# Expert stage: the gathered rows turned by a transposing DMA from the second tile on

## The reference

```python
def _moe2_ref(x, w_gate, w_output_gate, w1, w2):      # N=1792 tokens, D=768, E=8, F=1024
    logits = x @ w_gate
    e_idx = np.argmax(logits, axis=1)
    ...                                               # gate_w: softmax weight of the chosen expert
    for e in range(E):
        mask = e_idx == e
        h = np.maximum(x[mask] @ w1[e], 0.0)
        ye = h @ w2[e]
        out[mask] = gate_w[mask, None] * eom[mask, e, None] * ye
```

## Time and profile before

| | |
|---|---|
| median of 3 runs | 1143.07 us |
| the profiled execution, its own time | 1139.88 us |
| its span, first to last instruction | 1138.1 us |
| PE busy | 1100.3 us, 97% |
| DVE busy | 594.7 us, 52% |
| ACT busy | 425.9 us, 37% |
| POOL busy | 256.5 us, 23% |
| mean granted TensorE clock | 0.990 |
| DMA | 104.11 MB, mean 91 GB/s |

### The profile page before, as it was taken

The page is one execution under the profiler, slowest core; times in us unless marked ns, Lnnn a source line. Parts: engine busy times, 40 slices in busy tenths (PEclk is TensorE's granted clock), DMA queues, the critical chain, the costliest instruction groups (busy, mean ns, idle before and its releaser), DMA issues.

```text
span 1138.1 us, 17823 instructions
## 1 busy us (share of the span) xinstructions
PE 1100.3 (97%) x6617; PEld 573.3 (50%) x6618; DVE 594.7 (52%) x837; ACT 425.9 (37%) x631; POOL 256.5 (23%) x235
## 2 busy tenths in 40 slices
PE   7989999999999999999999999999898999999996
PEld 3434444444455555555555555556454555555554
DVE  7888888887433443333343300015656565556721
ACT  5768777777511111211111200001535253353510
POOL 4756767672200000000000000000211122112211
PEclk9999999999999999999999999999899999999999
DMA  5412222210121111111100501000848355366400
GB/s 144 122 49 62 61 65 58 66 25 17 60 67 56 56 55 55 55 55 55 55 28 1 195 28 41 28 32 23 296 163 319 118 211 206 108 217 225 142 20 18
DMA packets 71978, 104.11 MB, mean 91 GB/s; under 512 B 29310, under 2 KB 47870, under 8 KB 71920
## 3 DMA queue, kind: packets, MB, share of 16 engines
q1 hardware_dynamic: 63680, 89.84, 24.0%
q0 software_dynamic: 3120, 11.02, 2.7%
q10 hardware_dynamic: 5120, 2.48, 0.8%
HBM read 93.88 MB, written 13.76 MB: 95 GB/s over the span
## 4 chain that ended last, share of the span: by engine, by line
PE 87%; ACT 4%; DVE 4%; issue 2%; DMA 2%; ACTq 0%; POOL 0%; DVEq 0%; POOLq 0%; SPq 0%
PE ps L1434 29%; PE ps L1449 15%; PE ps L1528 12%; PE ps L1357 10%; PE ps L1506 7%; PE ps L1336 5%; PE ps L1316 2%; ACT arena L815 2%; DVE arena L1042 2%; PE ps L1348 2%; PE ps L1299 2%; PE ps L1338 1%; DMA arena<-in_moe_w 1%; PE ps L1515 1%; PE ps L1493 1%
## 5 line engine op out<-in xcount | busy, mean ns | idle before, releaser
L1434 PE MATMUL ps<-arena 128*128 128x448 f16 x1728 | 328.8, 352 | 0.0
L1434 PEld LDWEIGHTS ps<-arena 128*128 128x128 f16 x1728 | 168.1, 98 | 155.7
L1449 PE MATMUL ps<-arena 128*128 128x392 f16 (+1 forms) x1008 | 167.3, 329 | 2.4 <-DVE arena L1022 2.4
L1506 PE MATMUL ps<-arena 128*128 128x512 f16 x648 | 150.5, 388 | 5.6 <-DVE arena L1229 5.6
L1042 DVE SCALAR_TENSOR_TENSOR arena<-arena 128x768 f16<-128x768 f32 (+1 forms) x112 | 113.1, 1066 | 74.1 <-ACT arena L815 74.0
L1528 PE MATMUL ps<-arena 128*128 128x384 f16 x864 | 143.3, 326 | 4.0 <-DVE arena L1234 3.6
L1449 PEld LDWEIGHTS ps<-arena 128*128 (+1 forms) x1008 | 98.4, 98 | 70.4 <-DVE arena L1022 2.8
L1357 PE MATMUL ps<-arena 128*128 128x448 f32 x288 | 133.0, 573 | 0.0
L785 ACT ACTIVATE arena<-ps 128x448 f32<-128x448 f32 x48 | 26.1, 543 | 263.0 <-PE ps L1434 263.0
L1016 DVE SCALAR_TENSOR_TENSOR arena<-ps,arena 128x448 f32<-128x448 f32 x48 | 30.0, 624 | 176.0 <-PE ps L1434 96.1
L1528 PEld LDWEIGHTS ps<-arena 128*128 128x128 f16 x864 | 83.5, 98 | 58.6 <-issue 2.5
(11 more groups left out here) (170 smaller groups left out, 1078.7 us busy)
## 6 DMA issues: line engine op xcount, KB each, us to landing
arena<-in_moe_w SPq DMA_DIRECT2D x48, 512.0 KB, 6.3
arena<-in_moe_w SPq DMA_DIRECT2D x64, 384.0 KB, 3.9
arena<-in_qk SPq DMA_DIRECT2D x23, 448.0 KB, 3.5
y_parts<-arena SPq DMA_DIRECT2D x16, 384.0 KB, 2.3
arena<-in_v SPq DMA_DIRECT2D x48, 96.0 KB, 2.6
arena<-in_moe_w_out SPq DMA_DIRECT2D x12, 384.0 KB, 5.5
arena<-in_w_out_t SPq DMA_DIRECT2D x11, 384.0 KB, 3.1
arena<-in_moe_w_gate SPq DMA_DIRECT2D x10, 384.0 KB, 4.2
```

Source lines behind the costliest of these rows:

```text
L1434: last = nc.tensor.matmul(ps[:, 2 * (b % 2) + g, 0:S], up_w[s][:, g, c, wl], xt[:, b * KC + c, xl], start=(c == 0 and wl + xl == 0), stop= ...
L1449: last = nc.tensor.matmul(ps[:, 4 + 2 * s + h, 0:cols], gt[:, f, gl, bass.ds(t * 128, 128)], wo[:, f, wl, h, 0:cols], start=(f == 0 and gl ...
L1506: last = nc.tensor.matmul(ps[:, b, :], x_t[:, xl, c], w1_s[s][:, c, wl, b * 512:(b + 1) * 512], start=(c == 0 and xl + wl == 0), stop=(c = ...
```

## The change

From tile 1 on TensorE and VectorE no longer take part in turning the rows. ScalarE issues one transposing DMA for all twelve blocks, `x_rows` to `x_t`, after the second `Relu` of the tile before and ahead of `rows_done`. TensorE waits for that DMA (`x_turned`) before `up(g, 0)`, and the next gather waits for it too. Tile 0 is still turned by TensorE and VectorE.

```diff
 def gather(g):                                   # POOL
-    pool.wait_ge(rows_turned, turned)            # turned = g
+    pool.wait_ge(x_turned, turned)               # turned = 16 * g - 16
     nc.gpsimd.indirect_dma_start(out=x_rows, ...)
...
+def turn_rows(g):                                # ScalarE
+    read = 16 * g + 16 if isinstance(g, int) else act.to_reg(16 * g + 16)
+    act.wait_ge(route, ROUTE_DONE)
+    act.wait_ge(gathered, read)
+    act.dma_start_transpose(x_t.rearrange("p l c m -> p (l c) m"), x_rows).then_inc(x_turned, 16)
...
 def tile(e, s, before, first):                   # ScalarE, end of the loop over b
+                turn_rows(g + 1)
                 if is_at(g, 0):
                     split_high(e + 1, 1 - s, range(KC))
                 else:
                     rows_done(before)
...
 def tile(e, s, before, first):                   # VectorE, between the splits
-                rows_out(g + 1)
...
 def tile(e, s, before, first):                   # TensorE
     g = before + 1
-    pe.wait_ge(x_t_ready, g + 1)
+    if is_at(g, 0):
+        pe.wait_ge(first_x_ready, 1)
+    else:
+        pe.wait_ge(x_turned, 16 * g)
     up(e, s, g, 0, first)
     if not is_at(g, 0):
         turn_hidden(before, 0)
         turn_hidden(before, 1)
     up(e, s, g, 1, first)
-    turn_rows(g + 1)
```

More of the change, by code:

```diff
@@ L328, in attention_moe_moe_kernel @@
         rows_turned = sem("rows_turned")
-        x_t_ready = sem("x_t_ready")
+        first_x_ready = sem("first_x_ready")
+        x_turned = sem("x_turned")
         hid_sum = sem("hid_sum")
@@ L585, in gather @@
                 if not isinstance(g, int):
-                    read, turned, copied = pool.to_reg(16 * g), pool.to_reg(g), pool.to_reg(g + 1)
+                    read, turned, copied = pool.to_reg(16 * g), pool.to_reg(16 * g - 16), pool.to_reg(g + 1)
                     pool.wait_ge(route, ROUTE_DONE)
@@ L593, in gather @@
                     pool.wait_ge(gather_idx_ready, g + 1)
-                    wait(pool, rows_turned, g)
+                    wait(pool, rows_turned, min(g, 1))
+                    wait(pool, x_turned, 16 * (g - 1))
                     if is_at(g, 0):
@@ L1221, in _, with first_rows_out @@
             y_low(TT - 1, 1)
[L1223 to L1227, removed]
+            def first_rows_out():
+                dve.wait_ge(rows_turned, 1)
                 for l in range(2):
-                    last = nc.vector.tensor_copy(x_t[:, l].rearrange("p c m -> p (c m)"), ps[:, bank + l, :].bitcast(F16)[:, 0:DM])
-                last.then_inc(x_t_ready, 1)
+                    last = nc.vector.tensor_copy(x_t[:, l].rearrange("p c m -> p (c m)"), ps[:, 2 + l, :].bitcast(F16)[:, 0:DM])
+                last.then_inc(first_x_ready, 1)
             def turned_hidden(g, b):
@@ L1235, in turned_hidden @@
                     .then_inc(hid_t_ready, 1)
-            rows_out(0)
+            first_rows_out()
             split_low(0, 0, range(KC, PIECES))
@@ L1484, in _, with turn_first_rows @@
             down(TT - 1, 1, range(4, FC))
[L1487 to L1490, removed]
+            def turn_first_rows():
+                pe.wait_ge(gathered, 16)
                 for l in range(2):
                     for c in range(KC):
-                        last = nc.tensor.transpose(ps[:, bank + l, :].bitcast(F16)[:, c * 128:(c + 1) * 128],
+                        last = nc.tensor.transpose(ps[:, 2 + l, :].bitcast(F16)[:, c * 128:(c + 1) * 128],
                                                    x_rows[:, l * DM + c * 128:l * DM + (c + 1) * 128], ident)
@@ L1497, in up @@
             def up(e, s, g, b, first):
-                if b == 1:
-                    wait(pe, hid_ready, 2 * g)
+                wait(pe, hid_ready, 2 * g + b - 1)
                 for c in range(KC):
@@ L1550, in _ @@
             pe.wait_ge(route, ROUTE_DONE)
-            turn_rows(0)
+            turn_first_rows()
             over_experts(pe, tile)
```

## The result

The changed kernel is slower: 1161.65 us median (1160.39 to 1162.46, 4 runs) against 1142.9 us (4 runs), ratio 1.0166, 95% interval 1.0148 to 1.0183. The profiled execution has a span of 1158.6 us against 1138.1.

The account below looks back on a forecast made before the run. PE was taken as the bound, with 87% of the chain of waits. (D - 1.96) - 0.67 + (D + 0.1) - 6.0 = 2 D - 8.5 = +4.7 us at D = 6.6, median 1147.8 us; 8-in-10 range 1139.5 to 1195.

Parts of the forecast that it names:

- rival B: The DMA outlasts rows_down, so PE waits for x in every tile from 2 on: +53 us, 1196 us; chance 0.25.
- D: Time from when ScalarE may issue the transposing DMA until PE may go on; taken as 6.6 us, bounds 2.3 and 9.6.
- D hidden in ordinary tiles: In ordinary tiles rows_down covers the transposing DMA, with 7.0 to 7.2 us available, so PE does not wait for x.
- term of -6.0 us: Nine tiles (4, 5, 7, 9, 10, 12, 14, 16, 17) each gain PE's 0.67 us of turning x.
- Which work was on the path: Of PE's 12.1 us removed, ordinary tiles gain 0.67 us each; second tiles of experts 2 to 6 gain nothing.
- The form of the two odd places: Tiles 1 and 3 cannot hide the DMA: shifts of D - 1.96 = +4.6 us and D + 0.1 = +6.7 us.
- budget of 8.3: Cover in us for the DMA in the five second tiles; each us of D beyond it costs one there.
- Nothing but rows_done and the splits stand behind the issue: On ScalarE only rows_done and w2 splits follow the issue; rows_done waits 8.05 us for PE anyway, so issuing is free.
- No cost to others: No term for slowed transfers; weights landing later by sharing DMA engines was named only as a way to be wrong.
- C: The DMA's twelve blocks are served one after another, D is 17 us: +169 us, 1312 us; chance 0.10.
- A: Quick transfer: D between 2.3 and 4.2 us at tiles 1 and 3; 1139.2 us at D = 2.3; chance 0.21.
- estimate of 1.5 us of transfer: Transposing DMA's transfer by the skill's 261 GB/s, putting D near its lower bound in an idle stretch.

Follow-up runs that it names:

- no_turning: The kernel before with the transposes and copies of x left out from tile 1 on, nothing in their place: 1134.51 us, ratio 0.9917.
- pool_order: The changed kernel with POOL's copy of the scatter indices ahead of the gather that waits for the transposing DMA: 1161.87 us, ratio 1.0149.
- traffic_only: The kernel before plus 18 transposing DMAs of 384 KB between scratch buffers, whose result no engine needs: 1150.54 us, ratio 1.0072.
- small_packets: The changed kernel with ScalarE's DMA as a plain copy in 1536 pieces of 256 bytes, turning nothing: 1155.11 us, ratio 1.0102.
- early_tile3: The changed kernel, but in tile 2 ScalarE issues tile 3's DMA after eight w2 splits, ahead of six of w1: 1156.64 us, ratio 1.0123.

## Why the prediction was wrong

It had the direction, slower, and put the loss at 4.7 us; 18.8 us were measured. That 1161.65 us lies in the wide range is owed to rival B, for whose sake the range reached to 1195. The step that failed is "D hidden in ordinary tiles", with its term of -6.0 us.

- **Which work was on the path**: right. no_turning gave -8.6 us; ordinary tiles went to 16.5 us, and the second tiles' turning lay in the shadow of the chain over the splits. (36 copies are not 19.8 us of DVE, since all 38 are busy 19.3; nothing hangs on it.)
- **The form of the two odd places**: right, and they hold most of the loss, but not their sizes. Tile 1 had D = 6.4 against 6.6 taken. Its step grew by 5.8 us, not 4.6, since the gather itself landed 12.9 us after tile 0's start and not 11.6. The step after it grew by 0.5 us where 0.7 less was expected: the eighteen matmuls behind the longer pause took 6.94 us against 5.75, at a granted clock of 0.57 against 0.70, which I had counted at nothing. (In the other runs that wait for x there they took 5.4 to 6.8 us.) Tile 3 was released by the DMA 9.6 us after its issue, taken as 6.6. `rows_down` came at 887.07, 17.85 us after the earlier trace rows, where 10.7 was predicted: 2.8 from tiles 1 and 2, about 3.0 from D, and 1.4 from the wait for DVE behind the late `rows_done`.
- **"D hidden in ordinary tiles"**: this is the step that failed. I took one D for all tiles and named 9.6 only as a far bound that would hold everywhere. It did not hold everywhere, but in exactly the second tiles of experts 1 to 5 D was 9.3 to 10.7 us, beyond the budget of 8.3: the eight w2 splits free their buffers just before, so the load traffic is in the way. Between tiles 4 and 17 the term was -5.4 us and came out as +2.2. Of these 7.6 us, 5.1 are the waits for x ahead of tiles 7, 9, 12 and 14, and 1.4 are waits for DVE of 2.02 and 1.54 us in tiles 11 and 15 instead of 1.08; 0.8 are three ordinary steps of 16.7 or 16.8 us. The rule that each us beyond the budget costs one is roughly borne out: D of 9.3, 10.1 and 10.4 gave waits of 0.7, 1.5 and 1.7 us, and 10.7 only 1.2, since `rows_down` of that tile began 2.02 us late.
- **"Nothing but rows_done and the splits stand behind the issue"**: true of ScalarE, but POOL was read for its gathers only. The copy of the scatter indices stands behind the gather, and `rows_done` waits for it. I named what was queued behind the waiting instruction on one engine of two. What this cost the changed kernel is not known by itself, since pool_order shows no gain.
- **No cost to others**: I asked whether the weights would land later only as a way to be wrong. traffic_only puts it at some 3 to 5 us, an estimate, mostly at the awaited weights of tile 3.
- **Rivals**: B had the right mechanism for second tiles, and its +53 us was much too much since D was 3.7 to 6.4 us in twelve of the 18 tiles. The blocks are not served one after another, as C had it: alone the DMA takes 3.7 us, not 17. A's 2.3 us is not reached even by the plain copy, 2.6.
- The Trainium skill (DMA: Bandwidth & Descriptors, the table with the effective bandwidth of a transposing DMA) led to the estimate of 1.5 us of transfer. Alone, 384 KB in 3.7 us with its start is 106 GB/s, and the copy's 2.6 us 151; the page has 261 and more. No run separates the start from the transfer, but for a DMA of this size the measured 3.7 us decides. The Trainium skill's 1309 ns for one block (VectorE: DVE Perf Modes, the three transpose paths), taken twelve times in a row, is ruled out by the same 3.7 us.

What stays open: how the DMA engines take turns between a queue of 256-byte and one of 3 to 4 KB packets was not measured by itself, nor why the transposing form holds ScalarE's queue and takes the engines longer than a plain copy of equal packets. That both the packets and the form have their part is shown by small_packets; which part is the larger is not.

## What to carry to other kernels

Price a new DMA at each place where it stands, by what else the DMA engines do there, and by its packets and its form, not by its bytes. Ask also whom it slows: transfers that nobody awaits cost some 3 to 5 us here, because they delayed one that somebody did. When you add work to a kernel to measure something, look where that work itself lands: 2.65 us of clearing a buffer looked like a cost of DMA traffic. And when a wait is moved to another event, read every in-order queue that has such a wait in it, down to the last small copy; a change that gains only where cover is long and the engines are idle should be made only there.

## What was not expected of the hardware

- A transposing DMA of 384 KB within SBUF: 3.7 us alone, up to 10.7 us (13.4 in pool_order) beside weight loads. A plain copy: 2.6 alone, up to 8.4. Plain, in 256-byte pieces: 3.5 alone, up to 10.6. For the same bytes the three took 4.2%, 1.6% and 2.8% of the 16 engines' time over the execution.
- Issuing it took 1.3 to 1.5 us of ScalarE's queue alone and often, not always, 5.0 to 7.1 beside full loads: one that landed in 10.4 us was issued in 1.5. The plain forms took 0.47 to 0.53 (3 KB rows) and 0.60 to 0.70 (256-byte pieces) at the same places. ScalarE's next instructions waited behind it, as after 854.53 in early_tile3.
- ScalarE's queue ran ahead of its arithmetic: the DMA at 865.62 in the changed kernel was issued before the `Relu` that stands ahead of it began, at 866.27:

```profile
865.62 2.37 ACTq L837 DMA_TRANSPOSE arena<-arena  x1
866.27 0.58 ACT L857 ACTIVATE arena<-ps 128x512 f32<-128x512 f32 x1
```
